# An attention, routing, experts and dense layer kernel on one core: held first loads, output stores on two queues, and a routing stage rearranged over three engines

## What is computed

```python
scores = q @ k.T / 8                      # 8 heads of 64, causal window of 64 positions
x = softmax(masked scores) @ v            # x: [2304, 512]
noisy = x @ w_gate + log1p(exp(x @ w_noise)) * noise     # 8 experts
top2, and the softmax of the two logits as shares
y[n] = sum over the two experts e: share * (relu(x[n] @ w1[e]) @ w2[e])     # 512 -> 1024 -> 512
h = y @ w_in                              # 512 -> 2048
g = h where h >= 1, 0 where h <= -1, (h + 1)**2 / 4 between
out = g @ w_out
```

## Time and profile before

| | |
|---|---|
| Runs shown | 1098.91, 1098.46, 1094.33 us; median 1098.46 |
| Profiled execution | 1098.48 us, of which span 1096.20 us |
| TensorE busy | 1078.1 us, 98% of the span; 5904 matmul records |
| VectorE, ScalarE, GpSimd busy | 346.3, 346.3 and 386.5 us |
| Chain that ended last | TensorE 95%, VectorE 2%, ScalarE 1%, DMA 1% |
| Granted TensorE clock, mean | 0.989 of 2.4 GHz |

### The profile page before, as it was taken

One profiled execution on the slowest core, in us unless ns is written; L12 is line 12 of the kernel. 1 busy time (PEld: TensorE's weight loads), 2 busy tenths in 40 slices (PEclk: granted clock), 3 DMA queues, 4 the chain that ended last, 5 costly groups with the idle time before them and its releaser, 6 DMA issues.

```text
span 1096.2 us, 17734 instructions
## 1 busy us (share of the span) xinstructions
PE 1078.1 (98%) x5904; PEld 893.9 (82%) x5905; DVE 346.3 (32%) x683; ACT 346.3 (32%) x794; POOL 386.5 (35%) x302
## 2 busy tenths in 40 slices
PE   8999989999999999999999999999999999999997
PEld 6999558888888888888888887988888888888886
DVE  5888641112211221122211221333332233333221
ACT  4666212222222222222222221523334334335333
POOL 6322059558753719082644604940010001100000
PEclk8999889999999999999999999999999999999999
DMA  7775445996441513333332401240011103101001
GB/s 225 227 247 160 140 125 193 327 312 223 172 153 51 179 57 115 115 115 129 97 137 77 163 29 58 87 135 20 20 38 41 38 1 77 39 1 39 0 1 39
DMA packets 50479, 120.57 MB, mean 110 GB/s; under 512 B 7104, under 2 KB 12352, under 8 KB 49920
## 3 DMA queue, kind: packets, MB, share of 16 engines
q0 software_dynamic: 16688, 62.66, 17.6%
q1 hardware_dynamic: 21184, 34.72, 10.1%
q10 hardware_dynamic: 12560, 22.55, 6.3%
HBM read 87.14 MB, written 32.77 MB: 109 GB/s over the span
## 4 chain that ended last, share of the span: by engine, by line
PE 95%; DVE 2%; ACT 1%; DMA 1%; issue 0%; ACTq 0%; DVEq 0%
PE bank L1162 7%; PE bank L1164 7%; PE bank L1177 7%; PE bank L1179 7%; PE bank L1163 7%; PE bank L1178 7%; PE bank L1226 6%; PE bank L1228 6%; PE bank L1227 6%; PE bank L1219 6%; PE bank L1221 6%; PE bank L1220 6%; PE bank L1185 3%; PE bank L1043 3%; PE bank L1069 2%; PE bank L1146 2%
## 5 line engine op out<-in xcount | busy, mean ns | idle before, releaser
L420 POOL TENSOR_TENSOR Wl<-stage,Wh 128x2048 fp32r<-128x2048 f32 x36 | 165.8, 4607 | 3.0
L920 DVE COPY y_out<-bank 128x512 f32<-128x512 f32 x43 | 29.7, 691 | 363.6 <-PE bank L1179 363.6
L1162 PE MATMUL bank<-Wh,xT_h 128*128 x344 | 138.4, 402 | 0.9 <-issue 0.8
L1164 PE MATMUL bank<-Wh,xT_l 128*128 x344 | 134.5, 391 | 0.0
L1177 PE MATMUL bank<-Wh,hT_h 128*128 x344 | 134.0, 390 | 0.4 <-DVE hT_l L924 0.4
L1179 PE MATMUL bank<-Wh,hT_l 128*128 x344 | 134.2, 390 | 0.0
L1163 PE MATMUL bank<-Wl,xT_h 128*128 x344 | 133.8, 389 | 0.0
L1178 PE MATMUL bank<-Wl,hT_h 128*128 x344 | 133.8, 389 | 0.0
L958 DVE SCALAR_TENSOR_TENSOR bank<-bank,square 128x512 f32<-128x512 f32 x72 | 50.4, 699 | 254.9 <-ACT square L705 254.9
L676 ACT ACTIVATE hT_h<-bank 128x512 fp32r<-128x512 f32 x86 | 46.9, 596 | 259.2 <-PE bank L1185 259.2
L418 POOL CAST Wh<-stage 128x2048 fp32r<-128x2048 f32 x36 | 68.5, 1902 | 155.7 <-PE bank L1179 151.5
(11 more groups left out here) (163 smaller groups left out, 1729.2 us busy)
## 6 DMA issues: line engine op xcount, KB each, us to landing
stage<-w POOLq DMA_DIRECT2D x32, 1024.0 KB, 5.7
y_sorted<-y_out ACTq DMA_DIRECT2D x43, 256.0 KB, 2.1
x_in<-x_sorted ACTq DMA_DIRECT2D x39, 256.0 KB, 2.7
x_sorted<-gath_b SPq DMA_DIRECT2D x20, 256.0 KB, 6.1
x_sorted<-gath_a SPq DMA_DIRECT2D x19, 256.0 KB, 4.3
x_rows<-x_blk SPq DMA_DIRECT2D x36, 128.0 KB, 3.3
out<-stage SPq DMA_DIRECT2D x36, 128.0 KB, 2.4
k_ring<-kT SPq DMA_DIRECT2D x8, 512.0 KB, 6.3
```

The costliest lines, as they stand in the source:

```text
L420: nc.gpsimd.tensor_tensor(Wl[:, s, cols], stage[:, c % 2], Wh[:, s, cols], ALU.subtract).then_inc(w_ready, 1)
L1162: nc.tensor.matmul(H_ps[a][:], xT_h[:, u, k], high, start=(k == 0), stop=False)
L1164: mm = nc.tensor.matmul(H_ps[a][:], xT_l[:, u, k], high, start=False, stop=(k == KD - 1))
```

## The change

- SyncE waits for the last slice of block 0's k before it issues k and q of block 1. The router weights are issued ahead of the values.
- GpSimd spreads two steps at a time between its masks, and issues the first expert's first weight load after step 7's spread, ahead of the iotas.
- The last two low pieces move from steps 35 and 37 to behind the choice of the experts. Three fillers are put ahead of the last logits; the 28 fillers after them become 18.
- The slot is split by adding and subtracting `GRID` (its steps are 128 there), three instructions in place of five; `pair_slot` is written after the one-hots. `all_hi` and `io_lo` are rescaled to match. The product at L882 moves to ScalarE. Of the 36 one-hots VectorE makes 24 and GpSimd 12, and TensorE takes them in eight runs, in an order of its own, with 3 and 2 fillers between.
- Only tile 0 is transposed ahead of tile 0; tile 1 is transposed in its middle.
- In the last group each output bank is finished before the next. The second half of every output tile is stored from ScalarE's queue.

```diff
+GRID = 1.5 * 2.0 ** 30
-    PART = 2 * NT // 3
+    ON_DVE, ON_POOL = (8, 16, 20, 24), (30, 34, 36)
+        def half_tile(t, h):
+            at = Q * (t // 2) + S * (2 * (t % 2) + h)
+            return out[at:at + Q], o_out[Q * h:Q * h + Q, o_slot(t)]
...
+            sp.wait_ge(k0_loaded[2], 16)
             load_k(1)
             load_q(1)
+            sp.dma_start(w_gn[:, :, 0:E], w_gate...).then_inc(gn_loaded, 16)
+            sp.dma_start(w_gn[:, :, E:2 * E], w_noise...).then_inc(gn_loaded, 16)
             for b in range(B):
                 load_v(b, 1)
-            sp.dma_start(w_gn[:, :, 0:E], w_gate...).then_inc(gn_loaded, 16)
-            sp.dma_start(w_gn[:, :, E:2 * E], w_noise...).then_inc(gn_loaded, 16)
...
             for t in range(NT):
                 sp.wait_ge(o_copied, t + 1)
-                for h in range(2):
-                    at = Q * (t // 2) + S * (2 * (t % 2) + h)
-                    sp.dma_start(out[at:at + Q], o_out[...]).then_inc(o_stored[o_slot(t)], 16)
+                sp.dma_start(*half_tile(t, 0)).then_inc(o_stored[o_slot(t)], 16)
...                                                        (GpSimd)
-            spread(0)
+            for s in range(2):
+                spread(s)
             for mask, ... in (odd, even):
                 ...
-                spread(1 if count == ODD_CONSTANTS else 2)
-            spread(3)
+                if count == ODD_CONSTANTS:
+                    for s in range(2, 4):
+                        spread(s)
+            for s in range(4, 6):
+                spread(s)
...
-            for s in range(4, 6):
+            for s in range(6, 8):
                 spread(s)
+            load_raw(0, 0)
-            step(nc.gpsimd.iota(io_lo[:], pattern=[[1, P]], ...))
+            step(nc.gpsimd.iota(io_lo[:], pattern=[[-1, P]], ...))
...
+            pool.wait_ge(route, ROUTE_LOW)
+            for c in range(ON_DVE[-1], 2 * NT):
+                inst = nc.gpsimd.tensor_scalar(oh_lo[:, c], io_lo[:], lo_f[...][:, c:c + 1], None, ALU.is_equal)
+                if c + 1 in ON_POOL:
+                    inst.then_inc(pool_onehots, 1)
...                                                        (ScalarE)
             first_k(slice(1, 2))
-            first_v(0)
             first_k(slice(2, 4))
-            for b in range(1, B):
+            for b in range(B):
                 first_v(b)
...
             nc.scalar.activation(all_hi[:], io_hi[:]...,
-                                 ACT.Copy).then_inc(route_act, 1)
+                                 ACT.Copy, scale=float(P)).then_inc(route_act, 1)
...
+            act.wait_ge(route, ROUTE_HIGH)
+            nc.scalar.activation(id_cols[:, 1], oh_hi[:], ACT.Copy, scale=io_p[:, 0:1]).then_inc(route_act, 1)
...
                 nc.scalar.activation(o_out[:, o_slot(t)], O_ps[o_slot(t)][:], ACT.Copy).then_inc(o_copied, 1)
+                act.wait_ge(o_copied, t + 1)
+                act.dma_start(*half_tile(t, 1)).then_inc(o_stored[o_slot(t)], 16)
...                                                        (VectorE)
-                if s >= 7 and s % 2 and s < 7 + 8 * PIECES:
+                if s >= 7 and s % 2 and s < 7 + 8 * PIECES - 4:
                     low_piece((s - 7) // 2)
...
+            for k in range(4 * PIECES - 2, 4 * PIECES):
+                low_piece(k)
...
-            then(nc.vector.tensor_copy(pair_slot[:], slot_f[:]))
-            then(nc.vector.tensor_scalar(slot_hi[:], pair_slot[:], 7, None, ALU.logical_shift_right))
-            then(nc.vector.tensor_scalar(slot_lo[:], pair_slot[:], P - 1, None, ALU.bitwise_and))
-            then(nc.vector.tensor_copy(hi_b[:], slot_hi[:]))
-            then(nc.vector.tensor_copy(lo_f[:], slot_lo[:]))
+            then(nc.vector.tensor_scalar(on_grid[:], slot_f[:], 0.25 - P / 2, GRID, ALU.add, ALU.add))
+            then(nc.vector.scalar_tensor_tensor(lo_f[:], on_grid[:], GRID, slot_f[:], ALU.subtract, ALU.subtract))
+            then(nc.vector.tensor_scalar(rest_f[:], on_grid[:], GRID, None, ALU.subtract))
...
-            nc.vector.tensor_scalar(id_cols[:, 1], oh_hi[:], io_p[:, 0:1], None, ALU.mult)
-            for c in range(2 * NT):
+            for c in range(ON_DVE[-1]):
                 inst = nc.vector.tensor_scalar(oh_lo[:, c], io_lo[:], lo_col[:, c:c + 1], None, ALU.is_equal)
-                if c % PART == PART - 1:
+                if c + 1 in ON_DVE:
                     inst.then_inc(onehots, 1)
+            then(nc.vector.tensor_copy(pair_slot[:], slot_f[:]))
...                                                        (TensorE)
+                if s == G + 4:
+                    keep_busy(banks[0], 3)
                 if s >= 6 and s % 2 == 0:
                     logits((s - 6) // 2)
-            keep_busy(banks[4], 28)
+            keep_busy(banks[4], 18)
             pe.wait_ge(route, ROUTE_PICKED)
...
             keep_busy(banks[4], 28)
-            for c in range(2 * NT): ...
+            pe.wait_ge(route_act, 5)
+            pe.wait_ge(onehots, 1);      find_tokens(0, 8)
+            pe.wait_ge(pool_onehots, 1); find_tokens(24, 30)
+            keep_busy(banks[4], 3)
+            pe.wait_ge(onehots, 2);      find_tokens(8, 16)
+            keep_busy(banks[4], 2)
+            pe.wait_ge(pool_onehots, 2); find_tokens(30, 34)
+            pe.wait_ge(onehots, 3);      find_tokens(16, 20)
+            pe.wait_ge(onehots, 4);      find_tokens(20, 24)
+            pe.wait_ge(pool_onehots, 3); find_tokens(34, 36)
...
+                        if isinstance(t, int) and t == 0 and a == 0:
+                            transpose_x(1, 1, 0)
...
-            for t in range(2):
-                transpose_x(t, t, 0)
-                keep_busy(banks[4], 6)
+            transpose_x(0, 0, 0)
+            keep_busy(banks[4], 6)
...
+                if g == BIGS:
+                    for u in range(BT):
+                        for f in range(FC - 2, FC):
+                            second(f, u)
+                else:
                     next_z(2); second(FC - 2); next_z(3); second(FC - 1)
```

More of the change, by code:

```diff
@@ L495, in _ @@
                                          pattern=[[1, E], [-1, E]], channel_multiplier=0))
-            for s in range(4, 6):
+            for s in range(6, 8):
                 spread(s)
-            step(nc.gpsimd.iota(io_lo[:], pattern=[[1, P]], base=0, channel_multiplier=0,
+            load_raw(0, 0)
+            step(nc.gpsimd.iota(io_lo[:], pattern=[[-1, P]], base=0, channel_multiplier=0,
                                 allow_small_or_imprecise_dtypes=True))
@@ L507, in _ @@
             assert n[0] == ALL_CONSTANTS
-            for s in range(6, G):
+            for s in range(8, G):
                 spread(s)
-                if s in (7, 10):
-                    load_raw(0, (s - 7) // 3)
+                if s == 10:
+                    load_raw(0, 1)
                 elif s in (18, 26):
@@ L1122, in _, with find_tokens @@
             keep_busy(banks[4], 28)
-            for c in range(2 * NT):
-                if c % PART == 0:
-                    pe.wait_ge(onehots, c // PART + 1)
-                mm = nc.tensor.matmul(ID_ps[:, 0:2 * TILES], oh_lo[:, c],
-                                      id_cols[:, :, :, c].rearrange("p a t -> p (a t)"),
-                                      start=(c == 0), stop=(c == 2 * NT - 1))
+            def find_tokens(first, after):
+                for c in range(first, after):
+                    mm = nc.tensor.matmul(ID_ps[:, 0:2 * TILES], oh_lo[:, c],
+                                          id_cols[:, :, :, c].rearrange("p a t -> p (a t)"),
+                                          start=(c == 0), stop=(c == 2 * NT - 1))
+                return mm
+            pe.wait_ge(route_act, 5)
+            pe.wait_ge(onehots, 1)
+            find_tokens(0, ON_DVE[0])
+            pe.wait_ge(pool_onehots, 1)
+            find_tokens(ON_DVE[3], ON_POOL[0])
+            keep_busy(banks[4], 3)
+            pe.wait_ge(onehots, 2)
+            find_tokens(ON_DVE[0], ON_DVE[1])
+            keep_busy(banks[4], 2)
+            pe.wait_ge(pool_onehots, 2)
+            find_tokens(ON_POOL[0], ON_POOL[1])
+            for k in range(2, 4):
+                pe.wait_ge(onehots, k + 1)
+                find_tokens(ON_DVE[k - 1], ON_DVE[k])
+            pe.wait_ge(pool_onehots, 3)
+            mm = find_tokens(ON_POOL[1], ON_POOL[2])
             mm.then_inc(ids_done, 1)
@@ L1257, in first, with second @@
                     dense_in(wide_bank(f)[:], f, zT_h, zT_l).then_inc(h2_done, 1)
-                def second(f):
+                def second(f, only=None):
                     pe.wait_ge(gl_ready, n + f + 1)
-                    for u in range(BT):
+                    for u in range(BT) if only is None else (only,):
                         if f == 0:
@@ L1269, in second @@
                             mm.then_inc(o_done, 1)
-                    if f < FC - 1:
+                    if f < FC - 1 and only is None:
```

(10 more changed lines are left out.)

20 lines of the change are left out of this document (11 added, 9 removed).

## The result

The changed kernel takes 1092.45 us in the median of 12 runs (1090.04 to 1093.64) against 1097.99 for the kernel before on the same chip: ratio 0.996, 95% interval 0.9948 to 0.9971, so 3 to 6 us less. I had forecast 1086.5, in a range from 1082.3 to 1090.8. That is 5.5 less by the medians and 6.0 by the profiled executions, about half of the 12.0 forecast.

What follows compares the result with a forecast made beforehand. TensorE's own instructions were taken as the bound, 95% of the chain of waits. Savings of 4.9 + 2.4 + 1.1 + 1.5 + 2.1 = 12.0 from 1098.48 gave 1086.5 us, range 1082.3 to 1090.8.

Steps and rivals of the forecast that it cites:

- Opening: From the first loads to attention block 4: holding block 1's k and q starts block 4 at 13.7; 4.9 us saved.
- the second transfers are the new limit, or the hold does little: Rival for the kernel's start: held transfers limit it or the key slice was late otherwise; 2 saved, 1089.4 us, chance 0.14.
- End of attention and first routing: Last logits to ranks: low-part subtractions moved off the path and fewer fillers let ranks start sooner; 2.4 us saved.
- my upper bound's case: Attention's end and first routing: clock stays high, logits take about 0.8, VectorE's 6.5 sets the time; 3.6 us saved.
- Slots and one-hots: From the ranks' end to the token ids: shorter slot split, one-hots shared with GpSimd, finds starting sooner; 1.1 us saved.
- GpSimd would be held off until VectorE was through: Rival in the routing's one-hots: GpSimd's twelve start only at 140.5, ids 1.6 late; 1088.1 us, chance 0.07.
- First tiles: From ids to the first expert tiles: tile 1's transposes and six fillers leave the path ahead of tile 0; 1.5 us saved.
- Stores: Kernel's end: output halves on two queues and tiles finished one by one issue the last stores sooner; 2.1 us saved.
- the parts do less than they say: Rival for the whole kernel: fillers, loads and clock give back everything but 2 to 5 us; 1095 us, chance 0.03.

Runs made afterwards that it cites:

- raw_first: The changed kernel with the first raw weight load issued before the spreads of steps 6 and 7 and the constants; 1088.41 us, ratio 0.9932.
- raw_by_sync: The changed kernel with the first raw weight load issued from SyncE's queue behind the noise instead of by GpSimd; 1087.96 us, ratio 0.9934.
- old_opening: The changed kernel with SyncE's and ScalarE's first transfers and GpSimd's program up to the second raw load as before; 1090.56 us, ratio 0.9939.
- no_hold: The changed kernel without SyncE's wait for the third key slice; 1093.75 us, ratio 0.9977.
- old_k_first: old_opening with the third key slice issued ahead of the first value transfer; 1089.36 us, ratio 0.9932.

## Why the prediction was wrong, and where it was right

**Opening, the step that failed.** The sentence was that the raw expert weight "now issued ahead of the iotas shifts with the blocks", among the edits costed at nothing. I had asked when the load would be issued in the program's order and not when it would land against the cast that stands between two steps' exponentials. The cast was due 3 us sooner, the load came 1.7 to 2.8 later, and the wait for it took back most of what had been won; raw_first and raw_by_sync, which move nothing but the load, return 3 to 4.5 (by the ratios and by the medians). The load was later because the spread of step 7 ended 0.9 to 1.7 later than before and because its issue then stood 0.8 to 1.1 longer. It was a wait that the kernel before did not show, because there the load just came in time (old_opening's cast waited 0.18): the question "what does the faster stretch reach next" was asked for q and k, and not for this queue.

A second term there was mis-sized. The key slice was to take 5.0 and land near 6.9; it took 7.64 and landed at 9.56 (6.3 in raw_first), SyncE's queue opened at 9.58 and not near 7, and block 4 began at 15.35, not 13.7. These 1.65 and the 2.3 of the wait are the 4.0 missing from the term. That the hold would do it was also mine: without it the slice took 5.2 (no_hold, old_k_first), and behind the first value 9.2 (old_opening). The runs show the place ahead of the first values doing it, and the hold doing nothing measurable. The rival "the second transfers are the new limit, or the hold does little", 0.14, was the nearest; its 1089.4 still assumed the load free.

**End of attention and first routing** was right in its sum, 2.38 for 2.4, by another road, so the agreement is luck. The clock stayed high: the 18 fillers took 4.04, not 6.9, and the choice and not the fillers released the ranks, which is my upper bound's case; but my 3.6 for it was too much. The choice came 0.9 sooner on the shifted time line, and cnt_gt then followed it 1.5 closer; the two low pieces, which I had put into a wait, outlasted the ranks by 0.3.

**Slots and one-hots** was wrong by 1.8. Up to the first eight one-hots the steps came as said (6.9 after cnt_gt, forecast 6.7). The first find came 0.3 later than said. The finds took 5.9 in all, 0.163 each, where I had 5.5 with the drain, from the 0.143 of weight loads alone; and the five fillers took 2.1 at the low clock instead of 1.1. The clock's part is luck of placing: unchanged code gave 14.46 to 15.47 from cnt_gt to the ids. Even the best of these is only 0.3 under the 14.80 of before, not 1.1, since the fillers (0.76) and GpSimd's share (0.49) ate the rest. GpSimd's comparison took 0.736, above the 0.65 up to which I had called it hidden; in the changed kernel it still held nothing up, since the twelve ended at 140.00 and the last finds began at 140.60, behind the slow fillers. The rival that GpSimd would be held off until VectorE was through did not come: GpSimd started at 131.17 and ran beside oh_hi and the one-hots. But in part the contention came: a comparison took 1.03 and 1.06 beside the two VectorE instructions with two SBUF inputs, 0.70 to 0.72 beside the one-hots, 0.60 alone, and VectorE's one-hots went from 0.165 to 0.174. "GPSIMD Engine Reference", Specifications, in the Trainium skill, names contention with instructions in a two-port mode or with two SBUF inputs: the trace agrees on those with two inputs, and no row here shows in which mode the one-hots ran.

**First tiles**: 0.93 for 1.5, the 16 fillers took 5.04 and not 4.46, at the low clock, and tile 0 starts 7.24 after the ids and not 6.6. **Stores**: 2.11 for 2.1, less the 0.14 found ahead of them, and most of it by the order and not by the queues.

The chances said faster by over 0.5% at 0.96; the ratio is 0.996, on the other side of that line, though its interval reaches both. I had given "the parts do less than they say" 0.03. Five terms that all had to land were each taken near their middle, and nothing was kept for a wait not yet in the trace.

## What to carry to other kernels

When a stretch is made faster, list every instruction that stands in program order inside it and belongs to other work, here a weight cast between two softmax steps, and compare the landing of its input with its new due time. Put a prefetch as early as its buffer allows, since a load that is just in time hides the next gain. And before work is shared out to a slower engine, check whether the consumer, not the producer, sets the pace: TensorE took the one-hots no faster than VectorE alone made them.

## What the runs showed that I had not expected

The issue of GpSimd's first weight load stood up to 4.05 us with no wait in the code there, in one place of the program only; it is not settled why. The same instructions of the routing took 14.46 to 15.47 us, by where TensorE's low clock happened to fall: in raw_first the five fillers between the finds ran at the high clock, in the changed kernel at the low one, 1.0 apart. A megabyte of weights took 5.55 us to land when issued at 22.66 and 8.8 when issued at 13.47 among the held transfers, and still came in time.
